# Order of work in slots 1, 13, 15 and 16 of a fused attention and two-MLP kernel

## The reference

```
phi(x) = concat(exp(p - m), exp(-(p - m)))   with p = x @ w_phi, m = max |p| over the 128 features
attention:  kv = phi(k)^T v;  z = sum of phi(k);  out = phi(q) kv / (phi(q) z + 1e-6)
first MLP:  u = x + real(fft over tokens and columns of x);  x = u + relu(norm(u) @ w1) @ w2
second MLP: x = x + relu((norm(x) * g) @ w1') @ w2'
```

## Time and profile before

| | |
|---|---|
| median of 3 runs | 1010.08 us (1009.77 to 1012.62) |
| the profiled execution | 1009.88 us |
| its span | 1008.1 us |
| TensorE busy | 994.5 us, 99% of the span |
| VectorE busy | 654.9 us, 65% |
| ScalarE busy | 556.9 us, 55% |
| GpSimd busy | 364.9 us, 36% |
| moved by DMA | 80.31 MB, 80 GB/s |

### The profile page before, as it was taken

How to read it: one execution, slowest core, us unless ns; L and a number is a source line. 1 busy time by engine, 2 the same in 40 slices (tenths; PEclk the granted TensorE clock), 3 DMA queues, 4 the chain that set the end, 5 groups by cost and what they waited for, 6 DMA issues and landing times.

```text
span 1008.1 us, 16789 instructions
## 1 busy us (share of the span) xinstructions
PE 994.5 (99%) x5868; PEld 920.5 (91%) x5868; DVE 654.9 (65%) x1156; ACT 556.9 (55%) x1018; POOL 364.9 (36%) x362
## 2 busy tenths in 40 slices
PE   8999999999999999999999999999999999999997
PEld 7999999999989999999899999998999999989996
DVE  5677777889966567565684656755577555765443
ACT  4565455664665565555655666556665656633431
POOL 3632333444351353422633327223172332622110
PEclk9999999999999999999999999999999999999999
DMA  6333331301253313223133232232314322242102
GB/s 173 80 78 72 72 72 36 71 13 34 62 153 100 84 63 95 66 93 105 44 93 88 70 105 63 73 106 64 95 63 140 102 78 79 63 146 63 63 2 63
DMA packets 101313, 80.31 MB, mean 80 GB/s; under 512 B 56944, under 2 KB 81776, under 8 KB 101232
## 3 DMA queue, kind: packets, MB, share of 16 engines
q1 hardware_dynamic: 100992, 78.91, 28.2%
q10 hardware_dynamic: 240, 0.33, 0.1%
HBM read 66.10 MB, written 4.72 MB: 70 GB/s over the span
## 4 chain that ended last, share of the span: by engine, by line
PE 93%; DVE 3%; issue 1%; ACT 1%; POOL 0%; DVEq 0%; ACTq 0%
PE bank L1180 39%; PE bank L1157 35%; PE bank L421 5%; PE bank L408 5%; PE bank L374 3%; PE bank L660 2%; PE bank L680 1%; PE bank L392 1%; PE bank L426 1%; PE bank L368 1%; PE bank L351 0%; ACT feat_k L499 0%; PE bank L331 0%; DVE xall L544 0%; DVE amax_k L470 0%
## 5 line engine op out<-in xcount | busy, mean ns | idle before, releaser
L1180 PE MATMUL bank<-w2op,hid 128*128 128x512 f32 x1728 | 423.3, 390 | 0.0
L1180 PEld LDWEIGHTS bank<-w2op,hid 128*128 128x128 f32 x1728 | 321.7, 188 | 53.4 <-issue 0.3
L1157 PE MATMUL bank<-x_T,w1op 128*128 128x384 f32 x1152 | 208.1, 335 | 0.0
L1157 PEld LDWEIGHTS bank<-x_T,w1op 128*128 128x128 f32 x1152 | 201.2, 188 | 3.9
L1157 PE MATMUL bank<-x_B,w1op 128*128 128x384 f32 x864 | 173.5, 336 | 0.0
L1157 PEld LDWEIGHTS bank<-x_B,w1op 128*128 128x128 f32 x864 | 154.4, 188 | 11.4
L1351 POOL TENSOR_TENSOR w_sums<-st_w 128x256 f32<-128x256 f32 x48 | 49.7, 1035 | 223.2 <-DVE w1op L1387 223.2
L1467 DVE SCALAR_TENSOR_TENSOR hid<-part_s,hid 128x384 fp32r<-128x384 f32 x141 | 98.2, 723 | 37.7 <-ACT hid L1463 37.5
L1319 POOL TENSOR_TENSOR x_sums<-xraw 128x256 f32<-128x256 f32 x30 | 22.3, 765 | 194.4 <-ACT xraw L1272 124.3
L1408 DVE TENSOR_TENSOR w2op<-st_w,w2op 128x1024 fp32r<-128x1024 f32 x48 | 62.8, 1307 | 45.9 <-ACT w2op L1404 45.9
L1463 ACT ACTIVATE hid<-part_s 128x384 fp32r<-128x384 f32 x141 | 73.3, 524 | 31.1 <-DVE part_s L1437 31.1
(11 more groups left out here) (181 smaller groups left out, 1505.4 us busy)
## 6 DMA issues: line engine op xcount, KB each, us to landing
st_w<-w1a SPq DMA_DIRECT2D x24, 512.0 KB, 3.4
st_w<-w2a SPq DMA_DIRECT2D x24, 512.0 KB, 3.7
st_w<-w1b SPq DMA_DIRECT2D x24, 512.0 KB, 3.4
st_w<-w2b SPq DMA_DIRECT2D x24, 512.0 KB, 3.7
v<-v SPq DMA_DIRECT2D x16, 256.0 KB, 3.9
out<-xall SPq DMA_DIRECT2D x16, 256.0 KB, 2.1
rawqk<-qkT SPq DMA_DIRECT2D x14, 288.0 KB, 4.1
rawqk<-qkT SPq DMA_DIRECT2D x14, 256.0 KB, 3.6
```

The costliest lines, as they stand in the source:

```text
L1157: last = nc.tensor.matmul(dst, w1op[g % 2][:, a, W1OP.index(w), c, :], xop[x][:, b, c, :], start=name in ("M2", "M1", "M7") and k_ == 0, s ...
L1180: last = nc.tensor.matmul(acc[t0 + t][:, :], hid[name, g % 2][:, x, P * t:P * (t + 1)], w2op[g % 2][:, y, j, :], start=first and k_ == 0, ...
```

## The change

- The warm products go from 10 to 9.
- Slot 1, TensorE: the third transpose moves from ahead of units 3 and 4 to between the second and third round of the kv products. ScalarE copies the first kv half ahead of that transpose's exponentials.
- Slot 13, ScalarE: the root goes from ahead of the last transposed exponentials to behind the kv copies.
- Slot 15, TensorE: unit 4 goes from behind P2 to right behind unit 3. ScalarE: the second Q copy goes ahead of the extra row, and both roundings of the fold go from ahead of the last transposed exponentials to behind the kv copies. VectorE: all of k's features go ahead of the difference and sum of P1 and P2 and of the fold's four steps, among which they were spread.
- Slot 16, ScalarE: the first rounding of x goes behind the transposed exponentials, and the second behind the kv copies.

```diff
--- before.py
+++ after.py
@@ -40,7 +40,7 @@
 DC = DM // P
 FP_ = FF // (2 * P)
 KH = DC // 2
-WARM = 10
+WARM = 9
 EPS = 1e-6
 
 
@@ -883,11 +883,12 @@
             pe_unit(pe, g, u)
         if g == 1:
             pe_transpose(pe, l, 1)
-            pe_transpose(pe, l, 2)
             pe_unit(pe, g, 3)
             pe_unit(pe, g, 4)
-            for r in range(3):
-                pe_kv(pe, l, r)
+            pe_kv(pe, l, 0)
+            pe_kv(pe, l, 1)
+            pe_transpose(pe, l, 2)
+            pe_kv(pe, l, 2)
             pe_num(pe, l, 0)
             pe_num(pe, l, 1)
             return
@@ -907,6 +908,8 @@
         pe_transpose(pe, l, 2)
         if g >= XT_SLOT:
             pe_unit(pe, g, 3)
+        if early:
+            pe_unit(pe, g, 4)
         if g == XT_SLOT:
             pe_xT(pe, 2)
             pe_xT(pe, 3)
@@ -916,7 +919,8 @@
             pe_stepB(pe, b_, "P2")
         if g < XT_SLOT:
             pe_unit(pe, g, 3)
-        pe_unit(pe, g, 4)
+        if not early:
+            pe_unit(pe, g, 4)
         if g == XT_SLOT:
             pe_xT(pe, 4)
             pe_xT(pe, 5)
@@ -971,18 +975,13 @@
         if g == PAIRS - 1:
             dve_first_sum(dve, "T3", xblock("B22"), xblock("B12"))
             dve_sumdiff(dve, b_, 0)
+            dve_features(dve, g, 1)
+            dve_sumdiff(dve, b_, 1)
+            dve_sumdiff(dve, b_, 2)
             dve_fold_odd(dve, *f_)
             dve_fold_even(dve, *f_)
-            dve_max(dve, g, 1, 0)
             dve_fold_lo(dve, *f_, True)
             dve_fold_lo(dve, *f_, False)
-            dve_shifted(dve, g, 1, 0)
-            dve_sumdiff(dve, b_, 1)
-            dve_sumdiff(dve, b_, 2)
-            dve_max(dve, g, 1, 1)
-            dve_max(dve, g, 1, 2)
-            dve_shifted(dve, g, 1, 1)
-            dve_shifted(dve, g, 1, 2)
             return
         dve_features(dve, g, 1)
         if g == XT_SLOT:
@@ -1018,8 +1017,8 @@
             act_q_copy(act, b_, 0)
         act_exp_qT(act, l, 1)
         if g == PAIRS - 1:
+            act_q_copy(act, b_, 1)
             act_exrow(act, *f_)
-            act_q_copy(act, b_, 1)
         if f_ is not None and g < PAIRS - 1:
             act_exrow(act, *f_)
         if a_ is not None:
@@ -1028,18 +1027,19 @@
         if g == 2:
             act.wait_ge(s_raw, 16 * 5)
             act_const_hi(act, "cs")
-        if g == STD_SLOT:
-            act_std(act, 0)
         if g == PAIRS - 1:
             act_q_copy(act, b_, 2)
-            act_fold_hi(act, *f_, True)
-            act_fold_hi(act, *f_, False)
         act_exp_qT(act, l, 2)
         act_kv_copy(act, l, 0)
         if g == XT_SLOT:
             act_xT(act, 2)
             act_xT(act, 3)
         act_kv_copy(act, l, 1)
+        if g == STD_SLOT:
+            act_std(act, 0)
+        if g == PAIRS - 1:
+            act_fold_hi(act, *f_, True)
+            act_fold_hi(act, *f_, False)
         if g == 2:
             for n in ("ss", "cd", "sd", "alt"):
                 act_const_hi(act, n)
@@ -1771,8 +1771,8 @@
             act_exp_k(act, 0)
             act_exp_qT(act, 0, 1)
             act_split_qk(act, 2)
+            act_kv_copy(act, 0, 0)
             act_exp_qT(act, 0, 2)
-            act_kv_copy(act, 0, 0)
             act_kv_copy(act, 0, 1)
             act_exp_k(act, 1)
             for g in range(2, PAIRS):
@@ -1780,12 +1780,12 @@
 
             l = PAIRS - 1
             act_place288(act, B - 2)
-            act_x_hi(act, 0, 0)
             for r in range(ROUNDS):
                 act_exp_qT(act, l, r)
-            act_x_hi(act, 0, 1)
+            act_x_hi(act, 0, 0)
             act_kv_copy(act, l, 0)
             act_kv_copy(act, l, 1)
+            act_x_hi(act, 0, 1)
             act_x_hi(act, 0, 2)
             act_x_hi(act, 0, 3)
```

## The result

The changed kernel takes **1012.72 us**, the median of 14 runs (1010.16 to 1014.05), against 1010.12 (1007.75 to 1012.62, 14 runs) for the kernel before beside it: a ratio of 1.0023, 95% interval 1.0014 to 1.0033. It is slower by 0.23%, which is less than the 0.3% that the prediction drew as its line, but the interval leaves out 1. The forecast of 1006.4, and its range up to 1008.2, were wrong. The profiled execution took 1013.84 us, 1012.0 of it span.

The account below looks back on a forecast made before the run. TensorE, busy nearly throughout, was taken as the bound, with VectorE also full from slot 14 on. From 1009.88 us, 4.5 won in slot 1 less 1.05 lost at S1 gave 1006.4, range 1003.0 to 1008.2.

Parts of the forecast that it names:

- the second rival: Slot 16: TensorE's 3.1 us idle drops the clock, kv takes 1.7 more, S1 is delayed 1.3; 1007.7 us, chance 0.18.
- S1's wait: Step S1, behind slot 16: TensorE waits over 1 us there, and what slots 13 to 16 save is given back.
- Slot 1, 4.5: Slot 1: units 3 and 4 hide under k's exponentials, output products start at 18.7 instead of 23.16; gain 4.5 us.
- the warm product's gain: Start of the kernel: one warm product fewer saves 0.3 us, between nothing and 0.44.
- Slot 13: Slot 13: with the root behind the kv copies TensorE's 1.43 us wait goes, but is given back at step S1.
- Slot 15, turns: Slot 15: VectorE's folds take turns with GpSimd's additions, so the finish starts at 237.9, 1.1 us later.
- that sign: Slot 15: even fold and odd rounding would each take over 1.5 us beside GpSimd.
- The first rival: Slot 15: folds meet GpSimd less or not at all, S1 2.5 early; 1002.9 us, halfway 1004.7, chance 0.25.
- The sum: Whole kernel: 4.5 us won in slot 1 less 1.05 lost at S1 is 3.45, giving 1006.4 us.
- the likeliest case: Whole kernel: the prediction's own case, 1006.4 us, 1005.7 to 1007.0 by its bounds, chance 0.48.
- The 1.05: Slots 15 and 16: the late finish makes the next finish start at 248.2 and step S1 come 1.05 us later.

Follow-up runs that it names:

- e5: The kernel before with the changes of slots 15 and 16 alone: 1019.07 us, ratio 1.0079.
- e9: The kernel before with the changes of slots 1 and 13, slot 16's kv products held for the first round of q's exponentials: 1014.13 us, ratio 1.0040.
- e2: The changed kernel with VectorE's order in slot 15 as before: 1007.42 us, ratio 0.9975.
- e8: The changed kernel with GpSimd's slot 15 additions held until VectorE has folded, and VectorE's second finish ahead of its T2 sum: 1005.61 us, ratio 0.9952.
- e1: The changed kernel with twelve unread identity products ahead of slot 16's kv products, filling TensorE's idle: 1003.86 us, ratio 0.9921.
- e6: The kernel before with the changes of slots 1 and 13 and the warm product alone: 1004.55 us, ratio 0.9937.
- e4: The kernel before with the change of slot 1 and nine warm products alone: 1005.22 us, ratio 0.9942.
- e7: The changed kernel with VectorE's old slot 15 order and six identity products ahead of slot 16's kv products: 1004.58 us, ratio 0.9935.
- e3: The changed kernel with GpSimd's additions of slot 15 held until VectorE's folds are through: 1008.23 us, ratio 0.9962.
- e10: The changed kernel with twelve identity products behind slot 16's kv products instead of ahead of them: 1010.65 us, ratio 0.9999.

## Why the prediction was wrong

**The step that failed** is the second rival, "the clock falls in slot 16", to which I gave a chance of 0.18 and a price of 1.7 us on the kv products, S1 1.3 later, 1007.7 in all. Both were wrong.

- *The chance.* The sum itself had 3.1 us of idle ahead of kv (measured 3.05), and the earlier trace rows had 3.16 followed by a clock of 0.54. Against it I had only "the idle is shorter", by 0.06. The rows spoke for the fall. It came in all 14 runs, in all of e5 and e9, and for idle of 1.4 us in half of e2's and of e8's.
- *The price.* I took the length of slot 1's fall, about 3.4 us, for that of any fall. There passes of 256 columns followed; here kv and output products of 65 and 130 do, and it lasted 20.48 us, 7.63 us of loss by e1. It ran past the output products, S0 and C0, so that S1's wait, which was to absorb a late kv, was used up: no idle stood ahead of S1 at 257.48, where e1 with its clock held waits 1.07.

The Trainium skill (TensorE: Matmul & The Clock Gate, "A second HAM failure mode: psum-queue depth-cycling") has frequent short idles between groups of products, in every round of a loop, as a cause of a clock that goes down and up between its two levels. Here a single idle of about 1.4 us went with a fall in half of e2's and e8's runs: short idles matter here too, but the repetition that the page tells of no run here shows.

**Right**, by the steps of the prediction:

- *Slot 1, 4.5.* Measured 4.09: output products at 19.07, forecast 18.7. The kv products wait 0.26 for k's exponentials (forecast 0.2), no idle of 3 us, full clock throughout, and v comes in time. Missing is the warm product's gain: the first projection took 2.34 us instead of 1.89, as the full clock came 0.85 later in that execution.
- *Slot 13.* The root is behind the copies and its wait gone. Of the 1.43 us, e6 shows 1.09 at the mark. I had said that all is given back at S1, where TensorE idles already; but the earlier trace rows has only 0.28 us of idle there, and in e6, with slots 15 and 16 as before, S1 came 1.09 earlier than in e4. S1 waits about 1 us only in kernels with slots 15 and 16 changed (1.07 in e1, 1.03 in e7). So this part of the path was wrong for slot 13 alone.
- *Slot 15, turns.* The even fold took 2.00 us and the small copy 1.59. I had named the odd rounding as the other long one; it ran free at 0.54, so that sign failed, but the sum did not: the finish started at 233.58, which with the 4.09 of slot 1 is 237.67, forecast 237.9. The kv products started at 239.72 so counted, forecast 239.85. The Trainium skill (SBUF — State Buffer, "SBUF: two separate sides") has the fp32 copy under the same lock as the folds, and 1.59 beside GpSimd against 0.15 without it agrees. The first rival, folds that don't collide, is out.
- *The sum.* With the clock held (e1) S1 started at 249.65 after 1.07 us of wait. Forecast were 249.57 (253.02 + 1.05 - 4.5) and over 1 us. The mark was at -3.36, forecast -3.45. So the sum of the likeliest case came out to 0.1 us for a kernel that never lets its clock fall, and this one isn't that. The 0.1 is in part luck. Slot 1 gave 4.0 to 4.1 us instead of 4.5 (e1's slot 2 starts its kv products at 26.15 against 30.11), and S1 came only 0.6 to 0.8 later instead of 1.05: two misses of opposite effect. The 1.05 doesn't follow from my own steps either: 237.9 and 10.34, less 2.3 and with 2.35, give 248.3 for the next finish, about 1.15 later.

Among the parts, the new order of slots 15 and 16 loses even at the full clock: e1's mark is 1.87 us behind e6's, with slot 2's kv products at the same time (26.15 and 26.12).

## What to carry to other kernels

Price an idle of TensorE's twice: once for itself, and once for all that runs behind it until the clock is back, which here was 20 us for an idle of 3. When a change makes a wait of 3 us in a trace that already shows one such wait with a slow stretch behind it, the fall is the main case and not a rival. If the idle can't be removed, a few products of no use in it are a cheap cure: twelve of them moved the mark from 4.27 us behind the kernel before to 3.36 ahead of it. A change that leaves the late part alone (e6) did as well without them.

## What the runs showed of the hardware

- The fall depends on chance where the idle is shorter: with 1.42 us (e2) and 1.39 us (e8) it came in half of the runs. It came in all eleven of e3, which pauses for 0.93 us in the middle of the kv products; that this pause alone is the cause isn't shown. With 0.65 and 0.56 us none of e6's five runs had it. The kernel before has the same two idles, and the falls of its slow runs aren't traced, so these aren't shown to be harmless.
- How long it lasts differs, by the profiled executions: 20.48 us in the changed kernel and e5, 17.07 in e2 and e9, 10.24 in e3, 6.83 in e10, 3.41 in slot 1 of the kernel before.
- In e9 the kv products ran at full clock for a while behind the idle; the records have the fall at 238.05, 1.7 us after they began, and half clock to 255.12. The clock can go down while TensorE is already at work again. So it did in e2, e3 and e10, 0.85, 1.86 and 1.77 us behind the end of the idle; in the changed kernel it fell within the idle.
- A VectorE copy of three columns can cost nearly as much as a GpSimd addition of 768 columns beside it (1.94 us): 1.59 us, against 0.15 without one.
